# Opening of a fused delta-rule attention kernel: the two halves of its inversion half a level apart on TensorE, fewer dummy products, and part of the weight casts on VectorE

## What is computed

```python
k_n = k / (np.linalg.norm(k, axis=-1, keepdims=True) + 1e-06)
for t in range(S):
    y[:, :, t] = np.einsum('bhd,bhde->bhe', q[:, :, t], state)
    v_old = np.einsum('bhde,bhd->bhe', state, kt)
    state = state + bt[:, :, :, None] * np.einsum('bhd,bhe->bhde', kt, vt - v_old)
```

## Time and profile before

| | |
|---|---|
| median of three runs | 1220.68 us (1217.96 to 1220.90) |
| the profiled execution's own time | 1219.58 us |
| its span, first to last instruction | 1217.8 us |
| mean granted TensorE clock over the span | 0.998 |
| TensorE busy | 1194.9 us, 98% of the span |
| VectorE busy | 694.0 us, 57% |
| ScalarE busy | 499.0 us, 41% |
| GpSimd busy | 579.1 us, 48% |
| opening step 0, to the gram of step 1 | 0 to 39.45 us |
| opening step 1 | 39.45 to 64.81 us |
| opening step 2 | 64.81 to 88.93 us |

### The profile page before, as it was taken

One profiled execution on the slowest core, in us unless ns is written; L12 is line 12 of the kernel. 1 busy time (PEld: TensorE's weight loads), 2 busy tenths in 40 slices (PEclk: granted clock), 3 DMA queues, 4 the chain that ended last, 5 costly groups with the idle time before them and its releaser, 6 DMA issues.

```text
span 1217.8 us, 29349 instructions
## 1 busy us (share of the span) xinstructions
PE 1194.9 (98%) x11601; PEld 1095.0 (90%) x11601; DVE 694.0 (57%) x1539; ACT 499.0 (41%) x1143; POOL 579.1 (48%) x590
## 2 busy tenths in 40 slices
PE   7999999999999999999999999999999999999997
PEld 3779999999999999999999999999968899989996
DVE  5665566766566676656666665653564845655000
ACT  5654433333443333344433434442214444444443
POOL 5773333333343433324343432422337877777764
PEclk9999999999999999999999999999999999999999
DMA  7351011011101101111110111002116431443110
GB/s 225 108 176 30 22 43 30 30 30 31 36 25 40 30 30 30 30 37 29 35 30 30 30 30 36 9 22 75 44 35 234 144 124 58 155 166 108 44 39 1
DMA packets 48247, 74.76 MB, mean 61 GB/s; under 512 B 7797, under 2 KB 36789, under 8 KB 48116
## 3 DMA queue, kind: packets, MB, share of 16 engines
q1 hardware_dynamic: 41396, 61.82, 15.7%
q0 software_dynamic: 6720, 11.07, 2.9%
HBM read 61.59 MB, written 12.65 MB: 61 GB/s over the span
## 4 chain that ended last, share of the span: by engine, by line
PE 92%; DVE 4%; DMA 1%; issue 1%; POOL 1%; ACT 0%; SPq 0%; POOLq 0%; DVEq 0%
PE ps L1330 27%; PE ps L1345 13%; PE ps L1570 6%; PE ps L1586 6%; PE ps L1195 4%; PE ps L1350 3%; PE ps L1575 3%; PE ps L1290 3%; PE ps L1590 3%; PE ps L1299 3%; PE ps L1220 3%; PE ps L1212 3%; PE ps L1223 2%; PE ps L1600 2%; PE ps L1297 2%; PE ps L1267 2%
## 5 line engine op out<-in xcount | busy, mean ns | idle before, releaser
L440 POOL TENSOR_TENSOR gl<-sg,gh 128x256 fp32r<-128x256 f32 x144 | 108.1, 751 | 392.0 <-ACT gh L994 391.9
L1330 PE MATMUL ps<-xh,wgh 128*128 128x256 f32 x864 | 263.9, 305 | 0.0
L1330 PE MATMUL ps<-xl,wgh 128*128 128x256 f32 x864 | 243.6, 282 | 0.0
L1330 PE MATMUL ps<-xh,wgl 128*128 128x256 f32 x864 | 242.9, 281 | 0.0
L664 DVE TENSOR_TENSOR MP<-ps,mE 128x512 f16<-128x512 f32 x126 | 87.0, 691 | 153.4 <-PE ps L1212 151.8
L1330 PEld LDWEIGHTS ps<-xh,wgh 128*128 128x128 f32 x864 | 163.9, 190 | 7.9 <-issue 7.0
L1330 PEld LDWEIGHTS ps<-xl,wgh 128*128 128x128 f32 x864 | 164.5, 190 | 0.0
L1330 PEld LDWEIGHTS ps<-xh,wgl 128*128 128x128 f32 x864 | 163.8, 190 | 0.0
L990 ACT ACTIVATE sg<-ps 128x256 f32<-128x256 f32 x144 | 55.3, 384 | 262.2 <-PE ps L1330 262.2
L947 ACT CAST Xs<-ps 128x512 f16<-128x512 f32 x126 | 73.6, 584 | 142.3 <-PE ps L1220 142.3
L1345 PE MATMUL ps<-woh,gh 128*128 128x392 f32 x288 | 109.0, 378 | 1.2 <-POOL gl L440 1.2
(11 more groups left out here) (215 smaller groups left out, 2651.9 us busy)
## 6 DMA issues: line engine op xcount, KB each, us to landing
W<-w_dram SPq DMA_DIRECT2D x16, 1536.0 KB, 11.0
betaT<-betaT_dram SPq DMA_DIRECT2D x48, 128.0 KB, 3.0
kin<-kv_dram SPq DMA_DIRECT2D x24, 192.0 KB, 2.7
kqT<-qT_dram SPq DMA_DIRECT2D x48, 96.0 KB, 2.6
vin<-kv_dram SPq DMA_DIRECT2D x24, 192.0 KB, 2.4
x_dram<-x2r SPq DMA_DIRECT2D x24, 192.0 KB, 2.0
woT<-woT_dram SPq DMA_DIRECT2D x1, 2304.0 KB, 8.6
stage<-w_gate_dram SPq DMA_DIRECT2D x6, 384.0 KB, 9.0
```

The costliest lines, as they stand in the source:

```text
L440: pool.tensor_tensor(gl[n % 2][:, :], gp[n % 2][:, :], gh[n % 2][:, :].bitcast(F32), ALU.subtract).then_inc(gl_ok, 1)
L1330: mm = pe.matmul(ps[n % 2][:, kind * TB:(kind + 1) * TB], w[:, kind, a, cs], v[m % 2][:, a, :], start=(a == 0 and x == 0), stop=(a == KT - ...
```

## The change

Three things change, all of them in steps 0 to 2.

On TensorE the second half's levels trail the first half's by half a level: half_masked of the next level stands directly behind half_products of the same half, and half_masked(1, 0) stands ahead of first_inverse(1). The dummy products in the levels of steps 1 and 2 go from 34 to 16 in each step, and none stands between the two halves' products any more.

On VectorE half_mask(1, 0) stands ahead of the norms and half_mask(1, 1) between norm_a and norm_b. ScalarE copies `Xs` and `XTs` of a half together, before those of the other half.

Of the six high parts of a group, ScalarE keeps pieces 6s and 6s+1. Pieces 6s+2 to 6s+5 go to VectorE: behind the masks of levels 3, 4, 5 and 6 in steps 1 and 2, and in step 0 behind those of levels 4, 5 and 6 and at the end of the step. They have a counter of their own, `whd_ok`.

```diff
--- before.py
+++ after.py
@@ -193,6 +193,7 @@
         "woe_hi", "woe_lo", "ones_ok", "ssq_ok", "rd", "ra", "hot_ok", "rank_ps", "cnt_ok", "slot_ok", "dif_ok", "exp_ok", "pay_ok", "id_ok", "tab_ok", "scat")]
     wexp = [sem(f"wexp{i}") for i in range(E)]
     w_ready = sem("w_ready")
+    whd_ok = sem("whd_ok")
     emb_in = sem("emb_in")
     rt_in = sem("rt_in")
     id_in = [sem(f"id_in{i}") for i in range(8)]
@@ -427,7 +428,10 @@
             pool.tensor_tensor(NL[:, hs, :], mNI[:, :].unsqueeze(1).to_broadcast([P, 4, P]), BA[:, 0, hs, :], ALU.subtract).then_inc(nl_ok, 1)
 
         def weight_low(n):
-            pool.wait_ge(wh_ok, n + 1)
+            if n % 6 < 2:
+                pool.wait_ge(wh_ok, 2 * (n // 6) + n % 6 + 1)
+            else:
+                pool.wait_ge(whd_ok, 4 * (n // 6) + n % 6 - 1)
             if n < NCG:
                 pool.tensor_tensor(wgt(wgl, n), staged(n), wgt(wgh, n).bitcast(F32), ALU.subtract).then_inc(wl_ok, 1)
             else:
@@ -759,6 +763,14 @@
             link(nc.vector.tensor_scalar(nx[:, 6, :], nx[:, 7, :], 1e-9, None, ALU.add))
             nc.vector.reciprocal(gate[:, 2 * m % B:2 * m % B + 2, 2 * m // B], nx[:, 6, :]).then_inc(pay_ok, 1)
 
+        def weight_high(n):
+            dve.wait_ge(w_in[n % NST], 16 * (n // NST + 1))
+            if n < NCG:
+                nc.vector.tensor_copy(wgt(wgh, n), staged(n)).then_inc(whd_ok, 1)
+            else:
+                dve.wait_ge(woe_ps, 1)
+                nc.vector.tensor_copy(wot(woh, n), staged(n)).then_inc(whd_ok, 1)
+
         def expert_high(e, c):
             dve.wait_ge(wexp[e], 32)
             cs = slice(c * PIECE, (c + 1) * PIECE)
@@ -860,16 +872,23 @@
             cg = s - 1 if s > 0 else None
             gram_masks(s, 0)
             gram_masks(s, 1)
+            half_mask(s, 1, 0)
             norm_a(s + 1)
+            half_mask(s, 1, 1)
             norm_b(s + 1)
             norm_c(s + 1)
             for l in range(1, LEVELS):
                 for hf in range(2):
-                    half_mask(s, l, hf)
+                    if l > 1:
+                        half_mask(s, l, hf)
                 if l == 2 and cg is not None:
                     state_update(cg)
                 if l == 4 and cg is not None:
                     x_low(cg)
+                if cg is not None and l > 2:
+                    weight_high(6 * s + l - 1)
+                elif l > 3:
+                    weight_high(l - 2)
                 if l == 6:
                     scaled_transposed(s + 1)
                     if s == 0:
@@ -878,6 +897,8 @@
             residual(s, 1)
             inverse_out(s, 0)
             inverse_out(s, 1)
+            if s == 0:
+                weight_high(5)
 
         for s in range(NS):
             (opening if s < PRE else body)(s)
@@ -952,7 +973,6 @@
             for hf in range(2):
                 wait(act, half_xx_ps[hf], (LEVELS - 1) * g + l)
                 nc.scalar.copy(half_cols(Xs, hf, l, 0), half_packed(bank_x[hf], l)).then_inc(half_xx_ok[hf], 1)
-            for hf in range(2):
                 wait(act, half_xts_ps[hf], (LEVELS - 1) * g + l)
                 nc.scalar.copy(half_cols(XTs, hf, l, 1), half_packed(bank_xt[hf], l)).then_inc(half_xts_ok[hf], 1)
 
@@ -1096,12 +1116,8 @@
                     keys_transposed(s + 1)
                 if cg is None and l in (2, 3):
                     expert_product(l - 1)
-                elif cg is None:
-                    weight_high(max(1, l - 2))
-                elif l > 2:
-                    weight_high(6 * s + l - 1)
-            if cg is None:
-                weight_high(5)
+                elif cg is None and l == 1:
+                    weight_high(1)
 
         for s in range(NS):
             if s == PRE:
@@ -1493,6 +1509,7 @@
             else:
                 expert_product(1)
                 expert_product(2)
+            half_masked(s, 1, 0)
             first_inverse(s, 1)
             if cg is not None:
                 outputs_y(cg, 2)
@@ -1500,8 +1517,9 @@
             else:
                 expert_product(3)
             for l in range(1, LEVELS):
-                half_masked(s, l, 0)
-                half_masked(s, l, 1)
+                half_products(s, l, 0)
+                if l == 1:
+                    half_masked(s, 1, 1)
                 if l == 5:
                     if cg is None:
                         pe.wait_ge(wet_ok, 2)
@@ -1509,9 +1527,9 @@
                 elif cg is None and l < 4:
                     expert_product(2 * l + 2)
                 else:
-                    warm(4, pA)
-                half_products(s, l, 0)
-                warm(1, pC)
+                    warm(2, pC)
+                if l + 1 < LEVELS:
+                    half_masked(s, l + 1, 0)
                 half_products(s, l, 1)
                 if cg is None and l < 3:
                     expert_product(2 * l + 3)
@@ -1521,8 +1539,10 @@
                     state_update(cg)
                 elif l == 3 and cg is not None:
                     y_transposes(cg)
-                else:
-                    warm(2, pC)
+                elif l + 1 < LEVELS:
+                    warm(2, pA)
+                if l + 1 < LEVELS:
+                    half_masked(s, l + 1, 1)
             warm(1, pC)
             half_residual(s, 0)
             warm(1, pA)
```

## The result

The changed kernel takes 1224.34 us (median of 22 runs, 1219.93 to 1228.11) against 1219.78 for the kernel before (22 runs, 1217.96 to 1221.55): ratio 1.0035, with a 95% interval of 1.0027 to 1.0044. It is slower by 4.6 us. I had forecast 14.8 more.

The account below looks back on a forecast made before the run. TensorE, with 92% of the chain, was taken as the bound; +3.4 (step 0), +1.2 (step 1's start), +5.1 and +5.1 (steps 1, 2) made +14.8, forecast 1235 us. Own range 1229 to 1240; with rivals 1217 to 1240.

Parts of the forecast that it names:

- rival A: Opening: VectorE gets in at every GpSimd boundary, each cast waiting for one instruction at most; +2.7, 1223 us; chance 0.14.
- The stagger, a level of 1.8: TensorE levels, steps 1 and 2: two half turns make 1.8 against 1.92, -0.6 a step over five levels.
- The step that failed: Opening: a VectorE cast waits for the running GpSimd instruction and the next one standing ready; cast 10 until about 63.4.
- residual +5.1: Steps 1 and 2: the residual starts 5.1 us later in each, at 66.95 against 61.89 in step 1.
- +3.4 for step 0: Step 0: the residual comes at 39.9 against 36.53, behind later norms, casts let in and low parts without a gap.
- The norms, keys 1.0 later: Opening: norms end 1.0 later, delaying GpSimd's keys and whole run by 1.0; level 2's mask gains 0.9 a step.
- Step 3 finds it no later than before and nothing is handed on.: Start of step 3: GpSimd's run ends 1.6 ahead of the gram, 68.1 against 69.9, so no delay passes on.
- Step 1's start, +1.2: Step 1's start: GpSimd's run holds `CT` until 5.0 + 0.65 behind the gram, against 4.45 before; +1.2.
- ScalarE holds up nobody: Levels: ScalarE loses four casts of 0.87 and has at most 1.6 of copies in a level of 1.8.
- Dummies cost nothing: Levels, steps 1 and 2: the dummies left take 0.33 for two and fit within the copy's 0.71.
- the clock 0 to +4, taken as 0 to 1: TensorE: gaps may bring the 1.2 GHz clock, 0.3 to 1.5 more a step; 0 to +4, taken as 0 to 1.
- A slip in the signs: Signs that would show the forecast right: gram of step 2 near 74.1 and of step 3 near 103.3.

Follow-up runs that it names:

- e9: Changed kernel with VectorE's fourth cast issued last in each step of the opening: 1221.7 us, ratio 1.0020.
- e13: Kernel before with the third stage's output DMA issued behind the pair of GpSimd hl instructions, not ahead of it: 1218.9 us, ratio 0.9997.
- e14: Kernel before with the third stage's pair of GpSimd hl instructions cut into four, the output DMA still ahead: 1221.6 us, ratio 1.0013.
- e5: Changed kernel with the norms ahead of both masks of level 1 again: 1220.1 us, ratio 1.0013.
- e4: Changed kernel with 15 dummy products (9 and 6) added in TensorE's two gaps at the start of step 3: 1221.6 us, ratio 1.0018.
- e6: Changed kernel with 4 dummy products in place of 2 in each half turn of the levels: 1220.3 us, ratio 1.0009.
- e1: Changed kernel with all six casts of a group back on ScalarE; stagger, norms and fewer dummies stay: 1220.4 us, ratio 1.0003.
- e2: Kernel before with only the four casts of a group moved to VectorE: 1221.9 us, ratio 1.0019.
- e10: Changed kernel with the casts back on ScalarE and 4 dummies in place of 2 in each half turn: 1222.1 us, ratio 1.0023.
- e16: Kernel before with low parts 2 and 3 of each group computed on VectorE: 1221.2 us, ratio 1.0013.
- e15: Kernel before with 4 dummies a level in place of 7 and nothing else: 1217.9 us, ratio 0.9991.
- e11: Changed kernel with norms ahead of both level 1 masks, 4 dummies in place of 2, and 6 and 4 dummies at step 3's start: 1225.1 us, ratio 1.0045.
- e3: Changed kernel with GpSimd's low parts made for 8 columns only, the products using the high parts instead: 1215.5 us, ratio 0.9960.

## Why the prediction was wrong

The direction held (slower), and 1224.3 lies in the range that took in rival A, but the forecast's own range began at 1229. That the 1223 of rival A comes near is luck. Its mechanism at the boundaries is the one that the runs show, but its sum had +1.5 in each of steps 1 and 2, which measured -0.7 and +0.6, and nothing in step 3 and behind it, where the loss came.

*The stagger, a level of 1.8.* Right for levels without a waiting cast, and more: 1.74. With the cast of 1.59 among them, the time from the first mask of level 2 to the end of the last one of level 6 is 8.8, where it was 8.5.

*The step that failed:* "such a cast waits for the GpSimd instruction that runs, and for the next one too if that stands ready directly behind it", and from it "it finds `kb` and low parts 8 and 9 ready behind that: it waits until about 63.4" for cast 10, and the wait of cast 11 for low part 10. Measured: cast 10 was issued at 58.46 and ended at 59.01, cast 11 issued at 60.20, inside `kb`, and ended at 61.23, ahead of low part 8. e9 shows the same for a cast issued in the middle of the low parts. The residual came even sooner than by rival A, which had put it at 63.45. In the place of "residual +5.1" in steps 1 and 2 stands -0.1 in step 1, and in the place of +3.4 for step 0 stands +0.3 at its end, with a slow stretch in it whose cost no run separates. I had carried one row from a place where GpSimd issues a DMA just ahead, to a place where it doesn't, and e13 and e14 show that this is the difference. The row on which I could have leaned in the opening, `CT` blocked by one low part, agreed with both readings. The Trainium skill, page "SBUF — State Buffer", section "SBUF: two separate sides", has the blocking for a whole instruction, and in the opening the trace agrees with it, instruction by instruction (e9: 0.69 and 2.15); in e14 the measurement differs from it, since VectorE waited through four.

*The norms, keys 1.0 later.* The keys start at 51.62, 2.0 later. 0.3 of it is the later gram; the two masks cost the 1.0 that I had (0.3 ahead of the norms, 0.7 between them); the other 0.7 is VectorE's `XTs` and `CT`, blocked at the step's start (0.93 for 0.42, 0.98 for 0.69), for which I had nothing. e5 takes part of it back, and some three microseconds with it.

*"Step 3 finds it no later than before and nothing is handed on."* It followed from the failed step: with each gram 5.1 later in its step, GpSimd would have been ahead. With the gram on time, GpSimd's low parts end at 93.0 in place of 89.3, and step 3 starts blocked. e4 prices this alone at 1.7, since its step 3 has the same blocking and no slow stretch (35.1 against 33.4); e6, with the smaller block, at 0.9.

*Step 1's start, +1.2.* `CT` ends at 44.08, 4.31 behind the gram, where it was 4.45. No loss there; what came instead is that `XTs` and the other half's `CT` are blocked too (0.93, 0.98).

*ScalarE holds up nobody.* e1 agrees from the other side: with the casts back, the same levels are slower (25.8 and 25.1 for 24.7 and 24.7).

*Dummies cost nothing; the clock 0 to +4, taken as 0 to 1.* The bounds held, the choice was low. The slow stretch costs 1.55 in step 3 (36.65 against the 35.1 of e4, which has the same waits; 1.6 and 1.5 in e2 and e10), and together with the waits 3.3. In the profiled execution that makes 1.9 of the 4.8 for the waits and the later gram, and 2.9 for the clock, if the 1.3 near 897 are counted with it. No edit reaches that place, and of two other profiles near the kernel before, e13 has no slow stretch there and e16 one of 6.8; so only the clocks of many runs show that the changed kernel is slowed more often. Of the 22 runs of the changed kernel 15 had a mean clock of 0.996 or less, of 138 runs of the kernel before 14. Four runs of the changed kernel at 0.997 have a median of 1220.3, 41 of the kernel before 1219.6: at that clock they differ by 0.7; the fastest run of each, 1219.9 and 1218.0, by 2.0. So of the 4.6, one to two are waiting and about three are clock. Why the clock falls more often is not shown. It isn't the number of dummies alone: e15 cut them at no cost. In the changed kernel doubling them gave back 4.1 (e6), with the casts on ScalarE it gave nothing (e10), and in e11 the slow stretches came in steps 1 and 2.

*Where the gain went.* Steps 1 and 2 together are no shorter (49.4 against 49.5): the turns of 0.87 would give 0.9 a step, but the cast that waits for `BA` takes 1.0 of it back, and the masks of level 1, ahead of the norms, are held up by the blocked start. e3 shows what takes it: with the low parts short, step 1 takes 23.0 and step 2 22.8, although casts still wait there (up to 1.21). The casts lengthen GpSimd's run (7.14 to 7.43) and the norms put it off by 2, and it then blocks VectorE at the next step's start.

*A slip in the signs.* By the forecast's own sum the grams of steps 2 and 3 stand at 64.81 + 9.7 = 74.5 and 88.93 + 14.8 = 103.7; it wrote 74.1 and 103.3. The time of 1235 doesn't rest on it.

What stays open: what decides in which step the clock falls. The stretch moves from place to place in kernels that differ little (step 3 in after, e2, e9 and e10; not in e1, e5, e6), and no single edit sets it. Where it falls is known from one profile of each kernel, how often only from the mean clocks of 5 to 22 runs.

## What to carry to other kernels

Before a wait is carried from one place of a trace to another, look at what the other engine did just ahead of it: here the same instruction waits for one GpSimd instruction in the opening, and for a whole run where that run stands behind a DMA issued by GpSimd. An engine that "nobody waits for" still takes turns at a shared port, so an edit that makes its run end later is paid by the first instruction of the next step. And where a change moves 3 us of work and the clock can take 1.6 by a single stretch, compare the clocks of the runs before explaining the time.

## What the runs showed of the hardware

VectorE's fp32 to fp32r cast of 128x768 takes 0.55 us alone, and GpSimd's subtraction of the same shape 1.8 us. Where both meet, the one that comes second waits for the running instruction, and the waiting one goes first at the boundary, even if the other's next instruction is ready (VectorE's cast of 64.00, GpSimd's third low part 2.15 for 1.8). Behind a DMA that GpSimd issues this did not hold: VectorE waited through four GpSimd instructions (3.39 us for 0.55), and moving the DMA behind the pair ended it.

TensorE, busy nearly without a gap since 95.83 and behind two waits of 1.13 and 0.89, was granted 1.2 GHz from about 98.3 on for 3.4 us, and the products of the gated layer took 0.41 in place of 0.28; the waits cost 1.7 (e4), the clock 1.55. In e10 a single wait of 0.77 stood ahead of the same fall.
